# The first 28 slots of the woven section laid out anew: four fills in their slots, two pairs turned later, three units' remainders on GpSimd

## What is computed

```python
def reference(q, k, v, w_gate, w_val, w_out, rms_g, w_in, w_out2):   # shortened; all float32
    # q, k, v: (8 batches, 8 heads, 576 tokens, 64); softmax attention inside chunks of 64 tokens
    scores = q_c @ k_c.T / 8;  attn = softmax(scores);  x = attn @ v_c     # -> x: (4608, 512)
    xn = x / rms(x) * rms_g
    h = silu(xn @ w_gate) * (xn @ w_val)        # 512 -> 1536
    y = h @ w_out                               # 1536 -> 512
    u = y @ w_in                                # 512 -> 2048
    g = u * clip(u + 3, 0, 6) / 6
    return g @ w_out2                           # 2048 -> 512
```

## Time and profile before

| what | us |
|---|---|
| median of 3 timed runs | 1653.3 |
| lowest and highest of them | 1642.41, 1655.88 |
| the profiled execution | 1644.85 |
| its span, first to last instruction | 1643.1 |
| TensorE busy in it | 1603.6 |

### The profile page before, as it was taken

One profiled execution on the slowest core, in us unless ns is written; L12 is line 12 of the kernel. 1 busy time (PEld: TensorE's weight loads), 2 busy tenths in 40 slices (PEclk: granted clock), 3 DMA queues, 4 the chain that ended last, 5 costly groups with the idle time before them and its releaser, 6 DMA issues.

```text
span 1643.1 us, 29732 instructions
## 1 busy us (share of the span) xinstructions
PE 1603.6 (98%) x11335; PEld 1568.2 (95%) x11337; DVE 1046.2 (64%) x1441; ACT 858.8 (52%) x1341; POOL 783.7 (48%) x774
## 2 busy tenths in 40 slices
PE   7899999999999999999999999999999999999998
PEld 5688999899999999999999999999999999999998
DVE  4878877868754446755454776665666865455454
ACT  4666766654644444644444565554655654434432
POOL 2543442459876564423240377777676631231231
PEclk9999999999999999999999999999999999999999
DMA  9777777644565655989987856647658986776674
GB/s 181 156 191 170 173 188 168 162 131 155 175 233 198 207 194 197 373 308 315 309 309 279 299 209 239 230 174 251 220 183 287 378 269 202 218 229 212 212 228 118
DMA packets 335646, 366.88 MB, mean 223 GB/s; under 512 B 186256, under 2 KB 299152, under 8 KB 332304
## 3 DMA queue, kind: packets, MB, share of 16 engines
q1 hardware_dynamic: 321584, 334.69, 64.8%
q0 software_dynamic: 8800, 28.85, 5.1%
q10 hardware_dynamic: 5120, 1.44, 0.5%
HBM read 200.80 MB, written 164.10 MB: 222 GB/s over the span
## 4 chain that ended last, share of the span: by engine, by line
PE 86%; SPq 4%; DMA 2%; DVE 2%; issue 2%; POOL 2%; ACT 2%; DVEq 0%; ACTq 0%; POOLq 0%
PE bx L989 14%; PE by L989 14%; PE by L990 14%; PE by L991 14%; PE bx L990 14%; PE bx L991 14%; DMA hl_b<-h_scratch 2%; SPq L583 1%; SPq L576 1%; PE att L958 1%; PE att L967 1%; PE att L914 1%; DVE tx L1523 1%; PE att L937 1%; SPq L590 0%
## 5 line engine op out<-in xcount | busy, mean ns | idle before, releaser
L989 PE MATMUL by<-tx,wr 128*128 128x384 f32 x840 | 285.4, 340 | 4.1 <-ACT vb L1201 2.5
L989 PE MATMUL bx<-tx,wr 128*128 128x384 f32 x840 | 285.5, 340 | 2.6 <-ACT gb L1201 1.2
L991 PE MATMUL bx<-tx,wr 128*128 128x384 f32 x840 | 281.0, 335 | 0.0
L991 PE MATMUL by<-tx,wr 128*128 128x384 f32 x840 | 280.9, 334 | 0.0
L990 PE MATMUL bx<-tx,wr 128*128 128x384 f32 x840 | 280.8, 334 | 0.0
L990 PE MATMUL by<-tx,wr 128*128 128x384 f32 x840 | 280.8, 334 | 0.0
L1574 DVE TENSOR_TENSOR hl_d<-hl_d 128x1536 fp32r<-128x1536 f32 x84 | 147.4, 1788 | 90.1 <-ACT hl_d L1273 90.1
L1892 POOL DMA_DIRECT2D out_dram<-ot x128 | 70.4, 558 | 248.1 <-DVE ot L1597 245.6
L1574 DVE TENSOR_TENSOR hl_b<-hl_b 128x1152 fp32r<-128x1152 f32 x84 | 117.5, 1414 | 106.7 <-ACT hl_b L1273 106.2
L1273 ACT ACTIVATE hl_d<-hl_d 128x1536 fp32r<-128x1536 f32 x84 | 123.3, 1486 | 112.6 <-DMA hl_d<-u_scratch 112.6
L989 PEld LDWEIGHTS by<-tx,wr 128*128 128x128 f32 x840 | 157.7, 188 | 7.6 <-issue 2.8
(11 more groups left out here) (200 smaller groups left out, 3769.6 us busy)
## 6 DMA issues: line engine op xcount, KB each, us to landing
hl_d<-u_scratch SPq DMA_DIRECT2D x84, 768.0 KB, 4.4
hl_b<-h_scratch SPq DMA_DIRECT2D x84, 576.0 KB, 5.8
u_scratch<-ut SPq DMA_DIRECT2D x48, 576.0 KB, 3.7
h_scratch<-ht SPq DMA_DIRECT2D x36, 576.0 KB, 3.5
u_scratch<-ub SPq DMA_DIRECT2D x96, 192.0 KB, 2.7
u_scratch<-ub SPq DMA_DIRECT2D x48, 384.0 KB, 2.5
h_scratch<-vb SPq DMA_DIRECT2D x72, 192.0 KB, 3.2
h_scratch<-vb SPq DMA_DIRECT2D x36, 384.0 KB, 3.1
```

Source lines behind the costliest of these rows:

```text
L989: pe.matmul(dst, w_hi, m_hi, start=start, stop=False, skip_group_check=not opens)
L991: return pe.matmul(dst, w_lo, m_hi, start=False, stop=stop, skip_group_check=not opens)
```

## The change

- The prologue turns pair 6 after the loop over the pairs and pair 7 after slot 1, both into `att`; scores of pair 6 come after the loop. The first product no longer waits for pair 7 to be turned but for the probabilities of pair 5 to be copied.
- ScalarE rounds unit 0 one iteration later; after the loop its list and that of VectorE are in a new order. Fills 2, 3, 5 and 4 of the first column block move to slots 0 to 3 on ScalarE (1 to 6 on VectorE), fill 6 from slot 8 to 9 and 10.
- Unit 1's sums get a buffer of their own (`w_sum_b`). Unit 0's second remainder goes from GpSimd to VectorE; the remainders of units 2, 3 and 5 go from VectorE to GpSimd (`LO_POOL_AT`).
- `XT3` comes in slot 2 instead of 4; the units 2 to 5 get new slots (`SUMS_AT`, `HI_AT`, `RAW_FIRST_AT`).
- The twelve pairs 6 to 17 get new slots; for all woven pairs `norm_rows` comes three slots after AT instead of four, many values of `AFTER` change, and `load_qk` of later pairs begins two slots earlier.
- On SP, `load_first_v(2)` and `load_raw_a(1)` come earlier; `load_qk(4)` and `load_raw_a(2)` come ahead of both `load_v`, and `store_x(0, 0)` stands between these two.

The diff, with unchanged lines kept only where the order matters:

```diff
+    w_sum_b = at("w_sum_b", [P, 3, 256], F32, TAIL + 18496)
...
-    QK_FIRST = {5: (5, 2), 6: (10, 2), 7: (27, 2), 8: (41, 2)}
+    QK_FIRST = {5: (0, 2), 6: (20, 4), 7: (30, 2), 8: (38, 1), 9: (57, 4)}
-        first, each = QK_FIRST.get(n2, (at_slot_of(2 * n2 - 4, SC) + 4, 1))
+        first, each = QK_FIRST.get(n2, (at_slot_of(2 * n2 - 4, SC) + 2, 1))
...
-        return NO * f + ((0, 2, 3, 4, 5, 1, 6)[o] if f == 0 else o) + 1
+        return NO * f + ((0, 1, 2, 3, 5, 4, 6)[o] if f == 0 else o) + 1
-    SECOND_FILL = {8: 0, 10: 1, 14: 2, 15: 3, 16: 4, 21: 5, 22: 6}
+    SECOND_FILL = {11: 0, 13: 1, 14: 2, 16: 3, 18: 4, 19: 5, 22: 6}
-        at_slot = SECOND_FILL if f == 1 else {4: 0, 10: 1, 11: 2, 16: 3, 18: 4, 20: 5, 22: 6} if f < 6 else {3: 0, 5: 1, 7: 2, 9: 3, 11: 4, 13: 5, 15: 6}
+        at_slot = SECOND_FILL if f == 1 else {4: 0, 11: 1, 12: 2, 15: 3, 16: 4, 19: 5, 22: 6} if f < 6 else {3: 0, 5: 1, 7: 2, 9: 3, 11: 4, 13: 5, 15: 6}
...
-            return w_raw_a[:, u % 2] if part == 0 else w_sum_a[:, :, :]
+            return w_raw_a[:, u % 2] if part == 0 else (w_sum_b if u == 1 else w_sum_a)[:, :, :]
...
-    EARLY = {6: (-6, -3, 1, 7), 7: (0, 3, 8, 12), 8: (7, 9, 14, 20), 9: (12, 15, 21, 24), 10: (18, 23, 26, 31), 11: (24, 28, 33, 37), 12: (32, 37, 39, 44), 13: (40, 43, 46, 50), 14: (45, 49, 52, 57), 15: (51, 56, 59, 63), 16: (58, 62, 64, 68), 17: (63, 68, 70, 76)}
-    AFTER = {7: 5, 8: 1, 11: 5, 12: 5, 25: 5, 20: 1, 24: 1, 33: 1, 29: 5, 30: 1, 15: 5, 17: 3, 18: 3, 23: 5, 32: 5, 28: 3, 13: 3, 26: 3, 16: 3, 22: 1, 34: 1, 19: 5, 21: 5, 27: 3}
+    EARLY = {6: (-6, -3, 2, 7), 7: (2, 7, 8, 12), 8: (8, 10, 15, 19), 9: (12, 15, 20, 26), 10: (18, 23, 29, 33), 11: (26, 29, 34, 37), 12: (32, 37, 38, 42), 13: (40, 44, 46, 49), 14: (46, 49, 53, 59), 15: (50, 54, 60, 63), 16: (56, 60, 65, 69), 17: (63, 67, 70, 76)}
+    AFTER = {7: 5, 8: 3, 11: 3, 12: 3, 25: 3, 20: 3, 24: 5, 33: 5, 29: 3, 30: 3, 15: 5, 17: 3, 18: 5, 23: 5, 32: 3, 28: 5, 13: 1, 26: 3, 16: 1, 22: 5, 34: 1, 19: 3, 21: 5, 27: 3, 9: 3, 6: 1, 14: 3, 10: 5, 31: 5}
...
-    FIRST_SUMS = {4: XT3, 9: XT4}
-    FIRST_HI = {3: 4, 8: 6}
-    FIRST_LO = {6: 4, 8: 6}
+    FIRST_SUMS = {2: XT3, 9: XT4}
+    FIRST_HI = {0: 2, 1: 3, 2: 5, 3: 4, 9: 6}
+    FIRST_LO = {1: 2, 3: 3, 4: 5, 6: 4, 10: 6}
-    RAW_FIRST_AT = {3: (0, 0), 4: (0, 8), 5: (1, 1)}
-    SUMS_AT = {2: (0, 1), 3: (0, 9), 4: (0, 12), 5: (1, 5), 6: (15, 9), 7: (15, 11), 8: (17, 1), 9: (17, 9), 10: (19, 1), 11: (19, 4)}
-    HI_AT = {2: ((0, 3), (0, 4)), 3: ((0, 9), (0, 10)), 4: ((1, 2), (1, 2)), 5: ((1, 9), (1, 11)),
+    RAW_FIRST_AT = {3: (0, 1), 4: (0, 12), 5: (1, 1)}
+    SUMS_AT = {2: (0, 1), 3: (0, 9), 4: (0, 13), 5: (1, 7), 6: (15, 9), 7: (15, 11), 8: (17, 1), 9: (17, 9), 10: (19, 1), 11: (19, 4)}
+    HI_AT = {2: ((0, 0), (0, 0)), 3: ((0, 10), (0, 11)), 4: ((1, 1), (1, 5)), 5: ((1, 8), (1, 9)),
-    LO_AT = {2: ((0, 6), (0, 6)), 3: ((0, 9), (0, 12)), 4: ((1, 4), (1, 4)), 5: ((1, 11), (1, 13)),
+    LO_AT = {4: ((1, 4), (1, 6)),
+    LO_POOL_AT = {2: ((0, 2), (0, 2)), 3: ((0, 11), (0, 12)), 5: ((1, 13), (1, 13))}
...
             if n > 3:
                 load_first(n, k, 1, k_loaded_first)
-            if n in (2, 4, 6):
+            if n in (2, 4):
                 load_first_v(n // 2 - 1)
-            if n in (5, 7):
-                load_raw_a((n - 5) // 2)
+            if n == 5:
+                load_raw_a(0)
+                load_first_v(2)
+                load_raw_a(1)
+        load_qk(4)
+        load_raw_a(2)
         load_v(NG)
+        store_x(0, 0)
         load_v(NG + 1)
-        load_qk(4)
-        store_x(0, 0)
-        load_raw_a(2)
         for m in range(0, 18):
             s, j = m // 3, m % 3
...
-        return bx[:, 0:2] if n % 2 == 1 else att[:, SB:SB + 2]
+        return bx[:, 0:2] if n < NG and n % 2 == 1 else att[:, SB:SB + 2]
...
-                pe.wait_ge(probsT_copied, n - 1)
+                pe.wait_ge(probsT_copied, n - 1 if n <= NG else n)
...
-            if m == 0 and st == 0 and o < 2:
-                pe.wait_ge(*((q_transposed, NQ), (k_transposed, NQ))[o])
+            if m == 0 and st == 0 and o == 0:
+                pe.wait_ge(probsT_copied, S_FIRST)
...
         keep_busy(4)
         for n in range(S_FIRST):
             transpose_probs(n)
-            scores(n + 1)
-            turn_qk(n + 2)
+            if n < S_FIRST - 1:
+                scores(n + 1)
+            if n < S_FIRST - 2:
+                turn_qk(n + 2)
             if n > 1:
                 transpose_x(n - 2)
             attend(n)
-        keep_busy(2)
+        turn_qk(S_FIRST)
         transpose_x(S_FIRST - 2)
+        scores(S_FIRST)
         pe.wait_ge(attn_scaled, S_FIRST)
         keep_busy(6, att[:, AB, :])
...
-                    keep_busy(3, att[:, AB, :])
+                if m == 0 and slot == 1:
+                    turn_qk(S_FIRST + 1)
...
         act.activation(row_sum[:, 0, 0:1], half[:, 0:1], ACT.Exp).then_inc(table_ready, 1)
         copy_k(0)
         for n in range(S_FIRST):
-            copy_k(n + 1)
+            if n < S_FIRST - 1:
+                copy_k(n + 1)
             exponentials(n)
             if n > 1:
                 norm_rows(n - 2)
             copy_probsT(n)
             if n > 0:
                 mean_square(n - 1)
-            if n in (3, 4):
-                weight_hi(0, n - 3)
+            if n in (4, 5):
+                weight_hi(0, n - 4)
             if n == 5:
                 fill_hi(0, 0)
-        copy_k(S_FIRST + 1)
-        exponentials(S_FIRST)
+        mean_square(S_FIRST - 1)
         norm_rows(S_FIRST - 2)
-        mean_square(S_FIRST - 1)
         weight_hi(1, 0)
+        copy_k(S_FIRST)
+        weight_hi(1, 1)
         norm_rows(S_FIRST - 1)
         fill_hi_early(1)
-        fill_hi(0, 5)
+        exponentials(S_FIRST)
         copy_probsT(S_FIRST)
-        weight_hi(1, 1)
+        fill_hi_early(2)
         fill_hi(0, 1)
-        fill_hi_early(2)
-        fill_hi(0, 2)
-        fill_hi(0, 3)
+        copy_k(S_FIRST + 1)
         for m in range(B0):
             ph, s, j = m // 18, m % 18 // 3, m % 3
...
-                n = woven(m, slot, AT, 4)
+                n = woven(m, slot, AT, 3)
...
-            if u == 1 and part == 0:
-                dve.wait_ge(w_lo, part_no(0, 1))
+            if u == 0:
+                dve.wait_ge(w_lo, part_no(0, 0))
+            if u - 1 in LO_POOL_AT and part == 0:
+                dve.wait_ge(w_lo, part_no(u - 1, 1))
...
         copy_q(0)
         for n in range(S_FIRST):
             shift_scores(n)
-            copy_q(n + 1)
+            if n < S_FIRST - 1:
+                copy_q(n + 1)
             if n > 2:
                 evict_x(n - 3)
             if n > 0:
                 scale_attention(n - 1)
-        shift_scores(S_FIRST)
-        copy_q(S_FIRST + 1)
+        copy_q(S_FIRST)
         evict_x(S_FIRST - 3)
         scale_attention(S_FIRST - 1)
+        weight_lo(0, 1)
+        shift_scores(S_FIRST)
         fill_lo(0, 0)
         evict_x(S_FIRST - 2)
+        evict_x(S_FIRST - 1)
         weight_lo(1, 0)
+        weight_lo(1, 1)
         fill_lo_early(1)
-        evict_x(S_FIRST - 1)
-        fill_lo(0, 5)
+        fill_lo_early(2)
         fill_lo(0, 1)
-        weight_lo(1, 1)
-        fill_lo_early(2)
-        fill_lo(0, 2)
-        fill_lo(0, 3)
+        copy_q(S_FIRST + 1)
         for m in range(B0):
             ph, s, j = m // 18, m % 18 // 3, m % 3
...
-            if 0 < u < UA2:
+            if 1 < u < UA2:
...
+            if u > 0 and part == 0:
+                pool.wait_ge(w_lo, part_no(u - 1, 1))
...
         ones.then_inc(consts_ready, 1)
         inverse_rms(0)
         inverse_rms(1)
+        inverse_rms(2)
         sums(0)
-        inverse_rms(2)
+        inverse_rms(3)
         weight_lo(0, 0)
-        weight_lo(0, 1)
-        inverse_rms(3)
+        inverse_rms(4)
         sums(1)
-        inverse_rms(4)
         inverse_rms(5)
         x_sum_early(XT1)
+        x_sum_early(XT2)
         x_sum(0, XT1)
-        x_sum_early(XT2)
         x_sum(0, XT2)
         for m in range(B0):
...
+                for u, part in parts_at(LO_POOL_AT, m, slot):
+                    weight_lo(u, part)
```

## The result

| | before | changed |
|---|---|---|
| median of 15 runs each, us | 1649.98 (1642.41 to 1655.88) | 1642.48 (1639.37 to 1651.61) |
| profiled execution, its time / span, us | 1644.85 / 1643.1 | 1639.71 / 1637.9 |
| its mean granted clock of TensorE | 0.997 | 0.998 |

The ratio is 0.9957, 95% interval 0.9944 to 0.9970: 7.5 us on the medians, 5.2 us on the two profiled spans. A second set of runs of the same two kernels gave 1640.6 against 1647.58, ratio 0.9964 [0.9947, 0.9980]. So the change makes the kernel faster by about 0.4%, within the 1% that the prediction called "within"; the forecast of 1647.3 was made on a median of 1653.3 from three runs, which fifteen runs put at 1649.98. Forecast: 6.0 us won. Measured: 5.2 by the spans, 7.5 and 7.0 by the medians.

The account below looks back on a forecast made before the run. TensorE was taken as the bound, so only its idle and low-clock time could be won: 1.5 + 0.9 + 3.6 = 6.0 us, from the 1653.3 median to 1647.3 us. The range was 1637 to 1657.5 us.

Parts of the forecast that it names:

- Step a: Prologue: rounding unit 0 later removes the 4.96 us hole; slot 0 an estimated 1 us earlier, not entered in the sum.
- Step b: SP's queue: v of pair 6 lands at 52.8 us, so its attention can't start before; most of the prologue's gain is lost.
- rival on GpSimd: GpSimd's remainders hold `norm_rows` in steps 0 and 1: 3.3 us slower, 1656.6; VectorE may be stretched too; chance 0.18.
- Step c: Slot 4, behind the load, sums and rounding of unit 2: at 56.8 us against 58.74, 1.9 us earlier.
- Step d: Slot 7, behind `XT3` and fill 4: `XT3` can start at 57.6 us, and slot 7 comes at 60.9 against 64.67.
- Step e: Slot 8: GpSimd's remainders of unit 2 delay `inverse_rms(6)` to 64.2 us; slot 8 at 65.4, 1.5 us earlier.
- Step f: Slots 8 to 15: later turning of probabilities takes 0.9 us off; slot 15 then comes 2.4 us earlier.
- Step g: Later pairs, 79 to 360 us: scaling rows one slot sooner wins 3.6 us of 10.9 idle.
- The other one, SP's queue: Later pairs: earlier `load_qk` makes SP wait for transpositions; costed at nothing, or one to three slots if slack is gone.
- a sign of being wrong: TensorE: a granted clock of 0.50 anywhere after 46 us would show the prediction wrong.
- Hidden anyway: Slot 8 comes earlier but the next wait takes it back: 0 to -1.5 us, 1652.5; chance 0.22.
- Most waits go: Most of TensorE's waits go: 1.5 + 1.6 + 10.9 = 14.0 us won, 1639.3; chance 0.13.

Follow-up runs that it names:

- experiment on the prologue: Kernel before, with only unit 0 rounded one iteration later and GpSimd's sums and remainders behind `inverse_rms`: 1648.06 against 1649.54 us, ratio 0.9992.
- kernel with rows at four: Changed kernel with `norm_rows` four slots after AT again instead of three: 1648.31 against 1649.54 us, ratio 0.9993 to the kernel before.
- old places: Changed kernel with pairs 9 to 17 in their old slots and all of `AFTER` as before: 1653.88 against 1649.54 us, ratio 1.0024.
- `XT4` ahead: Changed kernel with unit 2's remainders on GpSimd in slot 4 and `XT4` ahead of them: 1638.13 us, ratio 0.9949 to the kernel before.
- eight and four: Changed kernel with unit 2's remainders and `XT4` in slot 4, unit 1's second remainder later, eight and four dummy matmuls: 1638.91 us, ratio 0.9955.

## Why the prediction was right, and where its steps failed

**Step a, right to leave slot 0 out of the sum.** Slot 0 moved by +0.4, -1.0 and -0.6 us where 1 us earlier was expected. The experiment on the prologue bears out the reason for leaving it out: there slot 0 came 3.6 us earlier, and slot 8 none the less 0.9 later. The waits of the prologue are no longer in one hole but in several of up to 2.5 us. The low clock there is not cured: it lasts 3.4 us in the profiled execution (42.6 to 46.0) and 6.8 and 10.2 us in the two others, against 6.8 before.

**Step b, right in its times, wrong in what they bind.** On SP's queue the issues came within about 1 us of the working, but for the start of `load_qk(4)` (37.8 instead of 35.0, in 8.7 us instead of 10.4). The third row was put at 51.76; `XT3` behind it was put at 57.6 and came at 57.42:

```profile
42.27 4.21 SPq L578 DMA_DIRECT2D qk_a<-in_k_dram  x8
...
47.61 1.28 SPq L612 DMA_DIRECT2D v_a<-in_v_dram  x2
...
51.88 0.72 SPq L620 DMA_DIRECT2D x_scratch<-xr  x1
```

But "the attention of pair 6 can't start before 52.8" was not the bound: slot 2 began at 55.50 behind VectorE, and the attention at 57.11. The step that failed is "on VectorE this lies beside TensorE's work, so I cost it at nothing". The rival on GpSimd had named the stretch (2.11 for 1.22) and put it at 8 us for nine of them, but set it beside the sum. TensorE waited 2.35 us for VectorE at slot 2, and slot 2 followed slot 1 by 4.54 us where it was 2.66. By the rows two things made that, and by the experiment with the remainders back on VectorE neither is the three units given to GpSimd: the stretching beside GpSimd's sums, which no run takes away alone, and the new order of VectorE's list, in which unit 1's second remainder stands ahead of the fills. The order alone is 1.4 us by the experiment on it; the prediction doesn't mention it.

**Step c, wrong.** Slot 4 at 60.46, 59.06 and 58.70 instead of 56.8. `sums(2)` began at 52.86, behind GpSimd's own sums of `x` and not at the landing, and took 4.1 us instead of 2.93: rows of 0.9 to 1.17 us where alone there is 0.72. In two of the three executions the clock was at 0.50 as well, from about 56.3 to 59.7 and 55.6 to 59.0.

**Step d, right in GpSimd, wrong on TensorE.** `XT3` ran at 57.42, and TensorE no longer waited at slot 7. It came at 63.62 and not 60.9, because TensorE itself was late from slot 2; in the other two executions at 62.19 and 62.05.

**Step e, right in its mechanism, too small.** The chain GpSimd, `norm_rows(6)`, transposition, slot 8 is the one forecast. `inverse_rms(6)` ends at 65.35 and 66.24 where 64.2 was reckoned, because the remainders' 4.17 us were prices of instructions that ran alone: they took 5.0 and 5.6, and `inverse_rms` another 0.7 more. Forecast -1.5 us at slot 8; measured -0.3, +0.9 and +0.9.

**Step f.** Slots 8 to 15 took 11.4 us in the profiled execution, 0.6 less than before (0.9 was forecast), and 12.5 and 12.4 in the others, where the clock was low for the first part. The total to slot 15 was forecast at -2.4 and was -0.9, +1.4 and +1.3. The kernel with rows at four, which in these slots differs little, had slot 15 at 76.16, but through slot 0 at 44.74: from slot 0 to 15 it took 31.42 us, as the changed kernel's profile did (31.40). That the slots themselves can be that much shorter was not seen.

**Step g, undersized, and by another way than it said.** Forecast 3.6 us of a bound of 10.9; measured 6.4 to 6.7 from slot 15 to 196. Of the 6.4, idle time gives 10.9 - 7.1 = 3.8, as forecast; the other 2.6 is less busy time for nearly the same instructions (2999 matmul records against 2972), spread over many rows, and I can't put it to a line. That the idle part agrees is in part luck. The step went at the 4.3 us for normalised rows, and these fell only to 3.6; what went is above all the 2.5 us of attention waiting for evicted rows and the 1.4 us for `vb`, less 2.0 that are new for a fill. The experiments say how it hangs together: the change without the sooner rows loses the waits for VectorE but has the rows late (9.2 us), and the rows a slot sooner bring that back to 3.6. Which part of the change took the waits for VectorE away isn't shown; with the old places the first is gone too, and 0.9 us of the second is left. The other way round, rows a slot sooner need the new places; without them the exponentials fall behind GpSimd's wait for a store. That is the first of the counterarguments in the step ("ScalarE waits for GpSimd itself, with snapshots queued behind"), with exponentials in place of snapshots. The other one, SP's queue, cost nothing: SP does wait for transpositions of the pair before, but TensorE never for `v`.

**What the total owes to luck.** Two misses cancel: the first slots were forecast 1.5 to 3.8 us too well, the later ones 3 us too badly. Some 2 to 3 us seem to go again behind slot 196: that stretch was 1299.4 us in the kernel before, 1301.5 to 1302.7 in three executions of the changed one. But the experiments, which change next to nothing there, lie between 1299.5 and 1307.7, and the two made from the kernel before at 1301.4 and 1301.5. So this is more likely the scatter of single executions, with the profiled one of before at its short end, than a cost of the change.

**The rivals.** GpSimd holding others was true in place (slot 8) and false in sign of the whole; with the remainders back on VectorE the kernel isn't faster. A spell of the low clock began after slot 0 in all three executions, for 3.4, 10.2 and 3.4 us, which the prediction had listed as a sign of being wrong. It is part of what the first slots lack; the kernel that had it at 1.00 from 46 to 79 us with dummies was 1.3 to 2.5 us faster at the most likely, and perhaps not at all, since the intervals overlap. "Hidden anyway" was true up to slot 15 and false behind it. "Most waits go" was not seen: 7.1 us of idle time stay from slot 15 to 196. One sum beside the rivals was loose: 1% faster, 16.5 us, would have taken over nine tenths of the 18.0 us idle from 46 to 360 us, not over half.

## What to carry to other kernels

Where GpSimd and VectorE both work on instructions with two SBUF inputs, price both at their stretched durations: here some 2.3 us on VectorE ahead of slot 2 (an estimate) and 1.5 us on GpSimd ahead of slot 8 stood in no term of the sum, at the two places where each was late. Taking away the longest hole of a trace is worth nothing where the next load or list is late anyway: 3.6 us won at slot 0 were gone by slot 8. Try it alone before building on it. When a wait shrinks less than a change wins, look at which other waits went. And a piece of work moved sooner in a woven order pays only together with the place of what it now stands in front of: either half of step g alone gave nothing or lost 0.25%, both gave 0.4%.

## What the runs showed of the hardware

Two-input instructions on VectorE and GpSimd stretch each other here. Three fills of 128x768, 2.85 us alone, took 3.60 and 3.56 us where the remainders were on VectorE or later, 5.13 and 7.18 us beside them, and 5.54 in the order with `XT4` ahead; GpSimd's sums of 128x256 went from 0.72 to between 0.91 and 1.17 us, and `inverse_rms`, one column wide, from 0.55 to 1.27. The Trainium skill (GPSIMD Engine Reference, Key points) says that the two share SBUF interfaces and contend when VectorE's instruction has two SBUF inputs; the trace agrees, and adds that GpSimd pays as well.

TensorE's granted clock fell to 0.50 (1.2 GHz) within or behind waits of 3.2 and 3.5 us ahead of slot 8, for 6.8 and 3.4 us, and within a wait of 4.0 us in the prologue experiment, for 6.8. In the changed kernel's own profile it fell at about 56.3 us behind a wait of only 2.35, for 3.4 us, while in another execution of the same kernel it stayed at 1.00 through the same wait of 2.3, and in the kernel before through one of 2.55. So the length of the last wait doesn't decide it alone. Whether a few dummy matmuls in the gap keep it up is not shown: with eight in each of two gaps it was 1.00 from 46 to 79 us, with eight and four it fell at 59.7, behind a wait of 2.0 at slot 4, and three kernels without the added ones (rows at four, old places, `XT4` ahead) had it at 1.00 from 46 to 79 us as well.
